# First products of the weights before the first scores: loads, term order, two subtractions and the visits of the first pairs moved in a fused attention and two-MLP kernel

## The reference, cut to what matters

```python
out_d  = attention(mean over groups of 4 rows of q, k, v), each row repeated 4 times
out_l  = attention(q, k, v) masked to |i - j| < 4
x      = (out_d + out_l) as (2304, 512)
x      = (((x @ w1) * (x @ w2)) @ w3) @ w_out          # d_ff 1024
y      = max(x @ u1, x @ u2, x @ u3) @ uo              # d_ff 768
```

## Time and profile before

| what | value |
| --- | --- |
| median of 3 runs | 704.42 us (703.98 to 704.64) |
| the profiled execution | 704.63 us |
| its span in the trace | 702.5 us |
| PE busy in the span | 689.5 us (98%) |
| DVE, ACT, POOL busy | 324.4, 229.7, 244.4 us |
| PE idle before its first instruction | 6.0 us |

### The profile page before, as it was taken

One profiled execution on the slowest core, in us unless ns is written; L12 is line 12 of the kernel. 1 busy time (PEld: TensorE's weight loads), 2 busy tenths in 40 slices (PEclk: granted clock), 3 DMA queues, 4 the chain that ended last, 5 costly groups with the idle time before them and its releaser, 6 DMA issues.

```text
span 702.5 us, 15420 instructions
## 1 busy us (share of the span) xinstructions
PE 689.5 (98%) x6686; PEld 615.4 (88%) x6686; DVE 324.4 (46%) x609; ACT 229.7 (33%) x493; POOL 244.4 (35%) x220
## 2 busy tenths in 40 slices
PE   5999999999999999999999999999999999999998
PEld 4777788888888888888887999999999999999998
DVE  3454554424554055432655335665616556155540
ACT  5365433313232223333655333212331113411212
POOL 5799432312234023241222147322641026401220
PEclk9999999999999999999999999999999999999999
DMA  9865222111222122103888473876516765256202
GB/s 313 278 219 156 64 88 76 57 43 55 77 77 68 32 77 71 59 26 112 315 312 318 172 285 145 302 287 249 201 61 224 274 235 212 88 210 224 90 1 90
DMA packets 25650, 109.67 MB, mean 156 GB/s; under 512 B 2928, under 2 KB 6256, under 8 KB 22128
## 3 DMA queue, kind: packets, MB, share of 16 engines
q1 hardware_dynamic: 25584, 108.70, 43.9%
HBM read 87.46 MB, written 21.23 MB: 155 GB/s over the span
## 4 chain that ended last, share of the span: by engine, by line
PE 91%; POOL 3%; DVE 2%; ACT 1%; issue 1%; DMA 1%; SPq 1%; ACTq 0%; DVEq 0%
PE psum L478 28%; PE psum L480 27%; PE psum L479 27%; PE psum L517 2%; PE psum L495 2%; PE psum L488 2%; POOL second_split L1021 2%; PE psum L526 1%; PE psum L505 1%; DMA attention<-ident 1%; ACT attention L864 1%; DVE attention L667 1%; POOL h_split L1021 0%; DVE gate L739 0%; SPq L409 0%
## 5 line engine op out<-in xcount | busy, mean ns | idle before, releaser
L1021 POOL TENSOR_TENSOR second_split<-xy,second_split 128x384 fp32r<-128x384 f32 x72 | 78.9, 1122 | 148.6 <-ACT second_split L864 148.6
L478 PE MATMUL psum<-x_split,weights_split 128*128 128x512 f32 (+1 forms) x320 | 120.4, 376 | 0.0
L480 PE MATMUL psum<-x_split,weights_split 128*128 128x512 f32 (+1 forms) x320 | 118.0, 369 | 0.0
L479 PE MATMUL psum<-x_split,weights_split 128*128 128x512 f32 (+1 forms) x320 | 117.9, 368 | 0.0
L1021 POOL TENSOR_TENSOR h_split<-gate,h_split 128x512 fp32r<-128x512 f32 (+1 forms) x40 | 47.1, 1177 | 201.7 <-ACT h_split L864 201.7
L478 PE MATMUL psum<-second_split,weights_split 128*128 128x384 f32 x324 | 108.4, 335 | 0.8 <-POOL second_split L1021 0.8
L480 PE MATMUL psum<-second_split,weights_split 128*128 128x384 f32 x324 | 108.2, 334 | 0.0
L479 PE MATMUL psum<-second_split,weights_split 128*128 128x384 f32 x324 | 108.2, 334 | 0.0
L478 PEld LDWEIGHTS psum<-x_split,weights_split 128*128 128x128 f32 x320 | 60.3, 189 | 11.2 <-issue 1.2
L480 PEld LDWEIGHTS psum<-x_split,weights_split 128*128 128x128 f32 x320 | 60.3, 189 | 10.3
L479 PEld LDWEIGHTS psum<-x_split,weights_split 128*128 128x128 f32 x320 | 60.4, 189 | 9.3
(11 more groups left out here) (98 smaller groups left out, 1217.0 us busy)
## 6 DMA issues: line engine op xcount, KB each, us to landing
weights_split<-units_split SPq DMA_DIRECT2D x27, 1792.0 KB, 7.3
units_split<-attention SPq DMA_DIRECT2D x18, 896.0 KB, 3.9
xy<-wa SPq DMA_DIRECT2D x40, 256.0 KB, 5.0
attention<-qk SPq DMA_DIRECT2D x16, 576.0 KB, 4.3
attention<-v_win SPq DMA_DIRECT2D x16, 384.0 KB, 3.5
attention<-v_down SPq DMA_DIRECT2D x16, 320.0 KB, 3.3
attention<-wb SPq DMA_DIRECT2D x18, 256.0 KB, 3.6
out_t<-spare SPq DMA_DIRECT2D x12, 192.0 KB, 1.9
```

The lines of the kernel that those rows point to most:

```text
L478: pe.matmul(out, lhs[:, 0], rhs[:, 0], start=first, stop=False, skip_group_check=read_between)
L479: pe.matmul(out, lhs[:, 0], rhs[:, 1], start=False, stop=False, skip_group_check=read_between)
L480: return pe.matmul(out, lhs[:, 1], rhs[:, 0], start=False, stop=last, skip_group_check=read_between)
L1021: return pool.tensor_tensor(out, full, high.bitcast(F32), ALU.subtract)
```

## The change

1. SP issues pieces 0 and 1 first, then q and k of pair 0, then pieces 2 and 3, then the mask. The rest of the written order stays.
2. Step 0 of the first half is issued whole at its first piece: four matmuls high by high, a wait for the low of `w_out` 0, four high by low, a wait for the low of `w3` 0, four low by high. The number of matmuls is the same.
3. The low parts of `w3` 0 and `w3` 1 are made by DVE (`early_low`, ahead of and behind `qk_sum(0)`), with a semaphore of their own, `w3_lo_early`; `w3_lo` counts from `w3` 2 on.
4. The visits of pair 0 move from S -0.5, T 7, V 12 to 3.5, 10, 14, those of pair 1 from S 15, T 22 to 16.5, 23.5; V of pair 1 stays at 31.9. Everything that `FOLLOWS` them moves too.

PE's order becomes step 0, S0, step 1, three pieces of step 2, T0, its last piece, three pieces of step 3, V0, its last piece, one piece of step 4, S1, the rest of step 4, step 5, T1, steps 6 and 7, V1. On SP the load of q and k for pair 1 now stands behind pieces 16 and 17. On POOL `v_sum(0)` stands before splits 6 and 7 (step 3) instead of before splits 4 and 5, and `v_sum(1)` behind splits 12 and 13 instead of before them. On ACT splits 14 and 15 stand before `copy_turned(1)`, and splits 4 and 5 before `exp_down(0)`.

```diff
+EARLY = 2
-FIRST_VISITS = {"S": [-0.5, 15, 34.5, 47.5], "T": [7, 22, 40.7, 53.7], "V": [12, 31.9, 45.3, 58.3]}
+FIRST_VISITS = {"S": [3.5, 16.5, 34.5, 47.5], "T": [10, 23.5, 40.7, 53.7], "V": [14, 31.9, 45.3, 58.3]}
...
+        def wait_w3(eng, m):
+            if m < EARLY:
+                eng.wait_ge(w3_lo_early, m + 1)
+            else:
+                eng.wait_ge(w3_lo, m - EARLY + 1)
...
-            load_qk(0)
             load_piece(0)
             load_piece(1)
+            load_qk(0)
             load_piece(2)
+            load_piece(3)
             sp.dma_start(mask, mask_in).then_inc(const_in, 16)
-            load_piece(3)
...
+            def first_product(i):
+                if i:
+                    return
+                high, both = (lambda i: w3_tile(0)[:, 0, P * i:P * (i + 1)]), w_out_tile(0)
+                pe.wait_ge(w_out_hi, 1)
+                pe.wait_ge(w3_hi, 1)
+                for i in range(4):
+                    pe.matmul(bank(i), high(i), both[:, 0], start=True, stop=False)
+                pe.wait_ge(w_out_lo, 1)
+                for i in range(4):
+                    pe.matmul(bank(i), high(i), both[:, 1], start=False, stop=False)
+                wait_w3(pe, 0)
+                for i in range(4):
+                    pe.matmul(bank(i), w3_tile(0)[:, 1, P * i:P * (i + 1)], both[:, 0], start=False,
+                              stop=False).then_inc(w3o_step, 1)
...
+            def early_low(m):
+                dve.wait_ge(w3_hi, m + 1)
+                low(w3_tile(m)[:, 1, :], stage_a[2 * m + 1], w3_tile(m)[:, 0, :]).then_inc(w3_lo_early, 1)
...
+                                 [(-3.5 + m, ("EARLY_LOW", m)) for m in range(EARLY)],
...
+            of_vector = [("SPLIT", 2 * m + 1) for m in range(EARLY)]
```

More of the change, by code:

```diff
@@ L328, in build @@
         w_out_hi, w_out_lo = sem("w_out_hi"), sem("w_out_lo")
-        w3_hi, w3_lo = sem("w3_hi"), sem("w3_lo")
+        w3_hi, w3_lo, w3_lo_early = sem("w3_hi"), sem("w3_lo"), sem("w3_lo_early")
         w12_hi, w12_lo = sem("w12_hi"), sem("w12_lo")
@@ L405, in load_piece @@
                     elif kind == "w3":
-                        sp.wait_ge(w3_lo, n + 1)
+                        wait_w3(sp, n)
                     else:
@@ L528, in values @@
                 mm.then_inc(down_filled, 1)
+            def first_product(i):
[13 more added lines that the diff above has]
+                              stop=False).then_inc(w3o_step, 1)
             def product(half, k, i):
                 m = F1 * half + k
+                if m == 0:
+                    first_product(i)
+                    return
                 if i == 0:
-                    pe.wait_ge(w3_lo, m + 1)
+                    wait_w3(pe, m)
                     if half == 0:
@@ L777, in make_y @@
                 add.then_inc(y_made, 1)
-            run = {"qk_sum": qk_sum, "down_max": down_max, "local_max": local_max, "scale_down": scale_down,
+            def early_low(m):
+                dve.wait_ge(w3_hi, m + 1)
+                low(w3_tile(m)[:, 1, :], stage_a[2 * m + 1], w3_tile(m)[:, 0, :]).then_inc(w3_lo_early, 1)
+            run = {"EARLY_LOW": early_low, "qk_sum": qk_sum, "down_max": down_max, "local_max": local_max, "scale_down": scale_down,
                    "scale_local": scale_local, "x_out": x_out, "W3O_OUT": product_low,
@@ L782, in _ @@
             for step in in_order(unit_jobs(["qk_sum", "down_max", "local_max", "scale_down", "scale_local", "x_out"]),
-                                 product_out(), after_parts("H"),
+                                 product_out(), after_parts("H"), [(-3.5 + m, ("EARLY_LOW", m)) for m in range(EARLY)],
                                  [(at, ("COMBINE", n)) for n, at in enumerate(preparations(0.5))],
@@ L1057, in _ @@
                    "E": lambda e, kp: split_y(0, e, kp)}
-            for step in in_order(unit_jobs(["v_sum"]), weight_splits(), x_splits(), after_parts("H"),
+            of_vector = [("SPLIT", 2 * m + 1) for m in range(EARLY)]
+            for step in in_order(unit_jobs(["v_sum"]), [x for x in weight_splits() if x[1] not in of_vector],
+                                 x_splits(), after_parts("H"),
                                  [x for x in first_activations(0.4) if x[1][0] == "E"]):
```

## The result

The changed kernel takes 706.76 us (median of 7 runs, 705.33 to 707.47) against 704.35 us (7 runs) of the kernel before: a ratio of 1.0028, 95% interval 1.0018 to 1.0037. It is slower by 2.0 us by the ratio and by 2.4 between the medians, outside the forecast's 703.1 to 706.2. The profiled execution took 706.78 us, its span 704.9.

The account below looks back on a forecast made before the run. PE was taken as the bound, busy 689.5 of 702.5 us. The front's gain goes to pair 1's load and v_sum(1), leaving V1 0.55 later: 705.2 for the profiled execution, median 705.0, range 703.1 to 706.2.

Parts of the forecast that it names:

- The mark: Start of pair 1's values (V1), at 40.24 before: what it gains or loses, the end gains or loses.
- The front: Start through S0: PE starts at about 5.05 instead of 5.98, step 0 ends at 9.9, S0 at 11.7.
- the two bounds: DVE's 512-column subtraction for a low part: about 0.7 us from below, up to 1.8 from above.
- The failed step: Before S1: q and k of pair 1 land at 23.8 instead of 22.4, late by the transfer of two pieces.
- the 1.7 us in hand: From step 2 to S1: PE reaches S1 at about 23.8, the same work 1.7 us earlier than before.
- One more term: Pieces 16 and 17 ahead of q and k of pair 1 delay that landing by 1.4 us.
- From S1 to V1: S1 starts at 25.9, ends at 27.75; PE waits 1.8 us before step 7; V1 starts at 40.8.
- two mechanisms that were to eat the gain: Load of pair 1 makes PE wait 2.0 us before S1; v_sum(1) is in the 1.8 wait before step 7.
- The issue wait: Inside S1: 0.76 us, taken as bound to a time, so passed free; rival that it stays, 705.7, chance 0.17.
- The surviving gain: Rival: q and k of pair 1 land by 21.8, S1 starts at 23.85; 703.0 to 703.7, chance 0.2.
- The falling clock: Rival: the wait before S1 drops matmuls to 1.2 GHz for 4.2 us, 2.1 more, 707.1; chance 0.05.

Follow-up runs that it names:

- e8: The kernel before with only positions moved (S1, T1, exp_local of pair 0; v_sum of pair 1 left at 18.5), no load changed: 703.64 us, 0.9990.
- e3: The changed kernel with v_sum of pair 1 back ahead of splits 12 and 13 on POOL: 705.02 us, 1.0013.
- e6: The changed kernel with q and k of pair 1 ahead of pieces 16 and 17 and v_sum of pair 1 ahead of splits 12 and 13: 705.11 us, 1.0013.
- e13: The changed kernel again, unaltered, for a second trace: profiled execution 708.31 us.
- e14: The changed kernel again, unaltered, for a third trace: profiled execution 707.21 us.
- e4: The kernel before with only the written load order of the changed one: 706.64 us, 1.0032.
- e11: The kernel before with only piece 0 ahead of q and k of pair 0: 704.28 us, 0.9989.
- e7: The changed kernel with a 4 KB read of q of pair 0 ahead of all other loads: 706.76 us, 1.0031.
- e2: The changed kernel with q and k of pair 1 loaded ahead of pieces 16 and 17: 706.62 us, 1.0031.
- e1: The changed kernel with the written load order of the kernel before: 705.34 us, 1.0017.
- e10: The changed kernel with old load order, pair 1's q and k ahead of pieces 16, 17, v_sum(1) ahead of splits 12, 13, both lows on POOL: 703.54 us, 0.9986.
- e12: The kernel of e8 run again for a narrower interval: 703.29 us, 0.9986.
- e9: The changed kernel with old load order, pair 1's q and k and v_sum moved ahead again, step 0 as four split products: 704.04 us, 0.9996.
- e15: The kernel before again, unaltered, for a second trace: profiled execution 705.41 us.

## Why the prediction was wrong

**The mark.** Right. The execution's time less V1 is 664.4 before, 664.1 after, 664.4 in e8. What V1 lost or won, the end did.

**The front.** Right on PE's start (4.75 for 5.05), wrong on the pace: all twelve matmuls of step 0 start 0.43 to 0.46 apart (5.46 us in all), so it ends at 10.2 and not 9.9; S0 waits 0.37 for q and k and takes 2.06 for 1.83. Step 1 then starts at 12.64, 0.9 later than forecast; in the old order it started at 12.29, with the same work behind it. The gain of the front was already nothing there. In e3, e6 and e13 the last four matmuls of step 0 were 0.23 apart, so this draw is one of the slower ones. The prediction called such a pace the level of 1.2 GHz; it is that pace, but the windows' granted clock reads 1.00 over this stretch, as it does over the start of the kernel before, so that the row of the clock does not show it. The lows of DVE took 1.21 and 0.92, between the two bounds, and the second ended at 12.59, just before step 1 at 12.64. It was not covered, as the prediction had it: with piece 3 at 11.0 (8.9 before) it became a wait of PE, of 0.63 us in e13 and 0.30 in e14.

**The failed step: when the loads land.** The prediction had "512 KB more ahead cost their transfer, 0.7 us a piece" and q and k of pair 1 at 23.8. They landed at 25.5, because the loads from q and k of pair 0 on were already late, piece 2 by 2.8 us and piece 15 by 1.75, before pieces 16 and 17 came in. The sum went by bytes ahead in the queue. The windows contradict that: up to 10.58 the changed kernel moved 247 GB/s, 2.6 MB, while piece 2, with all that stands ahead of it 1344 KB, landed only at 10.0. In the kernel before the same 1344 KB were there at 7.2, when 1.8 MB had moved. Bytes had gone by; the landing had not come. With both pieces ahead the time is 2.3 to 2.5 us longer in the kernel before too (e4), and four traces of the changed loads have it; one piece ahead does not cost it (e11). The slow executions of e4 have no trace, so that the lateness is shown in the changed kernel alone.

By the Trainium skill ("DMA: Bandwidth & Descriptors", Queues, rings and completion order) each pair of a queue and one of the 16 DMA engines is a ring of its own, and one load is split across up to 16 of its queue's rings. Landings that come late while the rate stays as it was (247 GB/s to 10.58, 262 before) agree with that. Which engine lags, and why behind two pieces, stays open: a small read of q and k ahead did not mend the time (e7).

The same lateness undid the other side of the sum, the 1.7 us in hand. The prediction had PE at S1 at 23.8; it was there at 26.48. Step 1 started 0.9 late, and as pieces 4 and 5 came late, so did their lows and, behind v_sum(0) on POOL, those of step 3: PE waited 0.63 before step 2, where nothing was forecast, and step 3 began at 20.82 in place of 18.6. Had q and k of pair 1 landed at 23.8, S1 would still have started at 26.5, not 25.9.

One more term was too small. Two pieces ahead of q and k of pair 1 were to cost 1.4 us. The landing is 2.8 later in e3 than in e2, which differ there in little else (24.3 and 21.5, with pair 0's at 7.0 and 7.1), and 1.8 later in e1 than in the kernel before.

**From S1 to V1.** Right to 0.03: 14.93 us (27.74 to 42.67) for 14.9, with the issue wait gone and 1.49 before step 7 for 1.8. Of the two mechanisms that were to eat the gain, v_sum before step 7 was there and near its size (the wait of 1.49 for 1.8; e3).

**The issue wait.** The prediction took it as bound to a time near 27.29. It is bound to a time and to a place, but the time is not fixed: it ended at 27.3, 27.4 and 28.1 in the kernel before, 28.85 in e2, 30.63 in e13, each time 2.4 to 2.8 us behind the start of a packet of the instruction queue. It is a floor under S1's end that makes early arrival worthless, and it took e2's gain. The Trainium skill ("Runtime: NRT & Kernel Launch", Instruction fetch mechanics) calls the crossing of a 16 KB block mostly hidden; if that is what PE stood for, here it was not, with waits of 0.2 (e10) to 2.3 us.

**The rivals.** The surviving gain had 0.2 and did not come. The falling clock had 0.05 and comes more often than that: of the changed kernel's seven runs two have a mean clock of 0.997, of e6's ten five have 0.998 (the medians of the two halves are 706.7 and 704.3), of 90 runs of the kernel before one; e2 and e7 have three each, e8 two, e3 and e12 one. It is no part of the median's loss, since the other five runs of the changed kernel have 706.66 as their median. The Trainium skill ("TensorE: Matmul & The Clock Gate", HAM oscillation) has waits for DMA between bursts do this. The rows of e7 and e13 agree, those of e2 (2.33 us) and of e3 (1.46 and 1.36 in S1, the clock at 1.00) show that it does not always come.

So the change lost by its loads and by v_sum. Of its parts the load order costs 2.3 to 2.5 us in the kernel before (e4) and 0.8 to 1.2 in the changed one (e1), v_sum of pair 1 behind splits 12 and 13 costs 1.1 to 1.5 (e3), and the term order and the two lows on DVE earn nothing that can be told (e9, e10). These do not add up, as the parts share the waits.

## What to carry to other kernels

When the first load of a full DMA queue is exchanged, take the landings of everything behind it as unknown until a trace shows them: here bytes ahead gave an early bound, not the landing. A gain at the front is worth what is left of it at the last wait before the dense stretch, so look there first; three waits behind the front were worth about 1 us by positions alone (e12). And a wait near 2 us on PE can have a price behind it too: the clock fell behind one of 1.97 us and not behind one of 2.33.

## What the hardware showed that was not expected

- 576 KB behind two loads of 256 KB took 4.2 to 7.7 us from issue to landing in eight traces (7.5 in the first of the changed kernel), in front of them 3.6 to 4.1.
- PE stood up to 2.33 us for "issue" in the middle of small matmuls (e2), 1.45 in a second trace of the kernel before (e15), and went on 2.4 to 2.8 us after the start of a packet of the instruction queue, in all ten traces that have the wait.
- The clock fell to 0.54 behind one wait of 1.97 us (e7) and to 0.72 behind waits of 1.28 and 1.66 close together (e13), while 1.38 and 2.33 (e2) left it at full.
- A DVE subtraction of 512 columns with both inputs in SBUF took 1.21 us, partly beside one of POOL's, and 0.92, partly beside another.
